# Weights' product first, and MoE blocks of 512 tokens in place of 384

## The reference

```python
# attention: q, k, v (2, 8, 768, 64), centroids (8, 16, 64)
q_assign = argmax(normalised q . normalised centroids); k_assign likewise
scores = where(q_assign == k_assign, scale * q @ k.T, -1e9)
attn = softmax(scores);  x = (attn @ v) as 1536 tokens x 512
# first MoE: w1, w2 (512, 1024), w3 (1024, 1024), w_out (1024, 512)
x = ((x @ w1) * (x @ w2)) @ w3 @ w_out
# second MoE: w_in (512, 2048), w_out (2048, 512), alpha (2048)
h = x @ w_in;  out = (max(h, 0) + alpha * min(h, 0)) @ w_out
```

## Time and profile before

| | us |
|---|---|
| median of 3 runs | 791.84 |
| lowest, highest | 790.97, 792.37 |
| the profiled execution | 791.99 |
| its span, first to last instruction | 790.2 |
| TensorE busy in the span | 761.5 |
| VectorE busy | 428.7 |
| ScalarE busy | 336.3 |
| GpSimd busy | 189.4 |

### The profile page before, as it was taken

The page is one execution under the profiler, slowest core; times in us unless marked ns, Lnnn a source line. Parts: engine busy times, 40 slices in busy tenths (PEclk is TensorE's granted clock), DMA queues, the critical chain, the costliest instruction groups (busy, mean ns, idle before and its releaser), DMA issues.

```text
span 790.2 us, 12079 instructions
## 1 busy us (share of the span) xinstructions
PE 761.5 (96%) x4290; PEld 712.8 (90%) x4290; DVE 428.7 (54%) x704; ACT 336.3 (43%) x679; POOL 189.4 (24%) x210
## 2 busy tenths in 40 slices
PE   5999999999999998899999999999999999999998
PEld 4887998898899987899999999999999999999997
DVE  5224988889889887542212115467344434443442
ACT  5124988888889787532112114242111112112111
POOL 2120576867767875300000000000000000000000
PEclk9999999999999999999999999999999999999999
DMA  8833464565555322330000003231010001001001
GB/s 284 163 100 98 101 155 105 127 142 127 121 126 134 92 66 63 85 108 1 1 1 0 0 0 107 80 121 67 0 41 1 1 1 40 0 0 40 1 1 40
DMA packets 63577, 54.13 MB, mean 69 GB/s; under 512 B 31264, under 2 KB 51760, under 8 KB 63536
## 3 DMA queue, kind: packets, MB, share of 16 engines
q1 hardware_dynamic: 63536, 53.59, 26.3%
HBM read 31.50 MB, written 3.19 MB: 44 GB/s over the span
## 4 chain that ended last, share of the span: by engine, by line
PE 75%; POOL 15%; issue 5%; DVE 2%; ACT 2%; DMA 1%; POOLq 0%; SPq 0%; ACTq 0%; DVEq 0%
PE slot L575 57%; PE acc L575 14%; POOL xf L520 3%; PE slot L638 3%; POOL xf L516 2%; POOL xl L526 2%; POOL v L469 1%; POOL oh L495 1%; POOL v L465 1%; POOL c L487 1%; POOL c L488 1%; PE slot L689 1%; POOL c L493 1%; POOL c L485 1%; DMA qk<-in_k 1%
## 5 line engine op out<-in xcount | busy, mean ns | idle before, releaser
L575 PE MATMUL slot<-xh,w 128*128 128x384 f32 (+1 forms) x1024 | 277.0, 336 | 0.0
L575 PEld LDWEIGHTS slot<-xh,w 128*128 128x128 f32 x1024 | 186.8, 188 | 2.4
L575 PE MATMUL slot<-xl,w 128*128 (+1 forms) x512 | 172.3, 336 | 0.0
L1027 ACT CAST gh<-gf 128x384 fp32r<-128x384 f32 x64 | 32.9, 514 | 204.2 <-PE acc L575 178.2
L1127 DVE TENSOR_REDUCE nm<-slot 128x1 f32<-128x768 f32 x96 | 91.2, 950 | 22.7 <-PE slot L575 22.3
L1133 DVE TENSOR_TENSOR pl<-slot,ph 128x384 fp32r<-128x384 f32 x192 | 97.6, 550 | 10.6 <-ACT ph L900 10.4
L900 ACT CAST ph<-slot 128x384 fp32r<-128x384 f32 x192 | 83.6, 487 | 35.9 <-PE slot L638 35.4
L575 PEld LDWEIGHTS slot<-xl,w 128*128 128x128 f32 x512 | 96.0, 187 | 2.2
L892 ACT ACTIVATE pf<-slot,nm 128x768 f32<-128x768 f32 x96 | 87.9, 916 | 8.8 <-DVE nm L1127 8.7
L575 PE MATMUL slot<-k,q 96*128 96x384 f32 (+1 forms) x384 | 83.6, 339 | 1.7 <-DVE xl L1089 1.7
L638 PE MATMUL slot<-ident,pf 128*128 128x128 f32 x576 | 81.5, 275 | 2.0 <-DVE pl L1133 1.6
(11 more groups left out here) (121 smaller groups left out, 1113.0 us busy)
## 6 DMA issues: line engine op xcount, KB each, us to landing
stage<-in_moe_w SPq DMA_DIRECT2D x16, 256.0 KB, 3.1
stage<-in_moe_w_in SPq DMA_DIRECT2D x16, 256.0 KB, 2.7
stage<-in_moe_w_out SPq DMA_DIRECT2D x16, 256.0 KB, 3.0
qk<-in_q SPq DMA_DIRECT2D x16, 192.0 KB, 3.9
...
```

Of the source, the lines that this page charges most:

```text
L575: return nc.tensor.matmul(o, a, b, start=start, stop=stop)
L1027: copy(gh[j % 2][:, :], gf[j % 2][:, :]).then_inc(gh_done, 1)
```

## The change

There are two parts.

1. The start: w3's first tile and w_out's first half megabyte are loaded first, q, k and v after the weights. TensorE turns w3 tile 0 and multiplies it chunk by chunk as the parts arrive (`product_first` waits for each part by itself), and the transposes of q and k, and the cluster scores, stand between the product tiles. The loop over tiles is written out. cn and al are turned in the acc banks, not in slot 0. ACT and DVE follow in the same order.
2. The MoE stages: a block is 512 tokens (`TN`), so there are three blocks and four output tiles in each. abh and abl are rings of four features (`NAB`) in place of eight; `ab_hi` waits for layer 2 of four features before. wch and wcl are halves of one tile. xh and xl are laid out chunk, token. The loops over the middle block are unrolled.

```diff
@@ -29,8 +29,9 @@
-NB = B * S // HS
-TB = HS // P
+TN = 512
+NB = B * S // TN
+TB = TN // P
@@ -42,6 +43,7 @@
+NAB = 4
@@ -108,8 +110,8 @@
-        xh = sb("xh", [P, NB * KC * HS], F32R)
-        xl = sb("xl", [P, NB * KC * HS], F32R)
+        xh = sb("xh", [P, KC * B * S], F32R)
+        xl = sb("xl", [P, KC * B * S], F32R)
@@ -163,25 +165,25 @@
-        asb = [sb(f"asb{i}", [P, HS], F32, ff) for i in range(2)]
-        ab = [sb(f"ab{i}", [P, HS], F32, ff) for i in range(2)]
-        wch = sb("wch", [P, NF, DM], F32R, ff)
-        wcl = sb("wcl", [P, NF, DM], F32R, ff)
-        abh = sb("abh", [P, NF, HS], F32R, ff)
-        abl = sb("abl", [P, NF, HS], F32R, ff)
+        asb = [sb(f"asb{i}", [P, TN], F32, ff) for i in range(2)]
+        ab = [sb(f"ab{i}", [P, TN], F32, ff) for i in range(2)]
+        wcx = sb("wcx", [P, NF, 2, DM], F32R, ff)
+        wch, wcl = wcx[:, :, 0], wcx[:, :, 1]
+        abh = sb("abh", [P, NAB, TN], F32R, ff)
+        abl = sb("abl", [P, NAB, TN], F32R, ff)
...
-        gh = [sb(f"gh{i}", [P, HS], F32R) for i in range(2)]
-        gl = [sb(f"gl{i}", [P, HS], F32R) for i in range(2)]
-        neg = sb("neg", [P, HS])
-        gf = [sb(f"gf{i}", [P, HS]) for i in range(2)]
+        gh = [sb(f"gh{i}", [P, TN], F32R) for i in range(2)]
+        gl = [sb(f"gl{i}", [P, TN], F32R) for i in range(2)]
+        neg = sb("neg", [P, TN])
+        gf = [sb(f"gf{i}", [P, TN]) for i in range(2)]
...
-        xview = lambda x: x[:, :].rearrange("p (n c t) -> p n c t", n=NB, c=KC)
...
-        pairs = lambda x: x[:, :].rearrange("p (b h c i t) -> p b h c i t", b=B, h=2, c=2, i=2)
+        xview = lambda x: x[:, :].rearrange("p (c n t) -> p n c t", n=NB, c=KC)
...
+        pairs = lambda x: x[:, :].rearrange("p (c i b h t) -> p b h c i t", b=B, h=2, c=2, i=2)
@@ -363,30 +365,33 @@
-            load_qk(0, 0)
-            load_v(0, 0)
-            load_v(0, 1)
-            load_qk(0, 1)
+            load_w3(0, 0)
+            load_wo(0)
...
-            load_w3(0, 0)
+            load_wo(1)
...
-            for i in range(NWO):
+            for i in range(2, NWO):
...
+            load_qk(0, 0)
+            load_qk(0, 1)
+            for parity in range(2):
+                sp.wait_ge(w3_turned, parity + 1)
+                load_w3(4 + parity, parity)
+            load_v(0, 0)
+            load_v(0, 1)
...
-            for parity in range(2):
-                sp.wait_ge(w3_turned, parity + 1)
-                load_w3(4 + parity, parity)
+            sp.wait_ge(w3_turned, 5)
+            load_w3(6, 0)
...
+            sp.wait_ge(w3_turned, 6)
+            load_w3(7, 1)
...
-            for parity in range(2):
-                sp.wait_ge(w3_turned, 4 + parity + 1)
-                load_w3(6 + parity, parity)
@@ -611,6 +616,8 @@
+                elif c == 1:
+                    pe.wait_ge(w3_lo, NF)
@@ -673,17 +680,14 @@
-                s = 2 - parity
-                if isinstance(f, int) and f < 4:
-                    source = stage[parity] if f < 2 else early[NWO + parity]
-                    if f < 2:
-                        pe.wait_ge(ld_stage[parity], 16)
-                    else:
-                        pe.wait_ge(ld_early[NWO + parity], 16)
+                s = 1 + parity
+                if f in (2, 3):
+                    source = early[NWO + parity]
+                    pe.wait_ge(ld_early[NWO + parity], 16)
...
-                    pe.wait_ge(ld_stage[parity], 8 * (f - parity))
-                if not isinstance(f, int) or f >= 2:
+                    pe.wait_ge(ld_stage[parity], 16 * (f // 2 + 1) if f < 2 else 16 * (f // 2))
+                if f >= 2:
@@ -699,40 +703,57 @@
+            def product_first():
...
+                o = slot[0][:, 0, :]
+                pe.wait_ge(piece_hi, 1)
+                pe.wait_ge(w3_hi, 1)
+                for g in range(2):
+                    mm(o, w3h[:, 0, g, :], woh[:, g, :], g == 0, False)
+                pe.wait_ge(piece_lo, 1)
+                for g in range(2):
+                    mm(o, w3h[:, 0, g, :], wol[:, g, :], False, False)
+                pe.wait_ge(w3_lo, 1)
+                for g in range(2):
+                    mm(o, w3l[:, 0, g, :], woh[:, g, :], False, False)
...
             def product_tile(f, parity):
...
-            for j in range(2):
+            turn_w3(0, 0)
+            pe.wait_ge(setup_act, 1)
+            nc.tensor.transpose(acc[0:D, 0, 0:P], cn[:, :], ident[:, :])
+            pe.wait_ge(ld_al, 16)
+            nc.tensor.transpose(acc[:, 1, 0:NJ], al16[:, :], ident[0:NJ, 0:NJ]).then_inc(cen_turned, 1)
+            product_first()
+            pe.wait_ge(piece_lo, 2)
+            product_wc(0, (2, 3))
+            turn_w3(1, 1)
+            for i in range(2, NWO):
+                pe.wait_ge(piece_lo, i + 1)
+                product_wc(0, (2 * i, 2 * i + 1))
+            turn_w3(2, 0)
+            pe.wait_ge(w3_lo, 2)
+            product_wc(1, range(NF // 2))
+            pe.wait_ge(table_done, 2)
+            for half in range(2):
+                turned(0, 0, half, True)
+            product_wc(1, range(NF // 2, NF))
+            for f in range(2, NF - 2):
+                turn_w3(f + 1, (f + 1) % 2)
                 for half in range(2):
-                    turned(0, j, half, True)
-            pe.wait_ge(setup_act, 1)
-            nc.tensor.transpose(slot[0][0:D, 0, 0:P], cn[:, :], ident[:, :])
-            pe.wait_ge(ld_al, 16)
-            nc.tensor.transpose(slot[0][:, 1, 0:NJ], al16[:, :], ident[0:NJ, 0:NJ]).then_inc(cen_turned, 1)
-            turn_w3(0, 0)
-            turn_w3(1, 1)
-            pe.wait_ge(table_done, 2)
-            for i in range(NWO):
-                pe.wait_ge(piece_lo, i + 1)
-                for f in range(2):
-                    if i == 0:
-                        pe.wait_ge(w3_lo, f + 1)
-                    product_wc(f, (2 * i, 2 * i + 1))
-            turn_w3(2, 0)
-            turn_w3(3, 1)
-            for half in range(2):
-                cluster(0, 0, half, True)
-            with pe.Fori(2, NF // 2) as i:
-                product_tile(2 * i - 2, 0)
-                turn_w3(2 * i, 0)
-                product_tile(2 * i - 1, 1)
-                turn_w3(2 * i + 1, 1)
-            for half in range(2):
-                turned(0, 2, half, True)
-            pe.wait_ge(w3_lo, NF)
+                    if f == 2:
+                        turned(0, 1, half, True)
+                    elif f == 3:
+                        cluster(0, 0, half, True)
+                    elif f == 5:
+                        turned(0, 2, half, True)
+                product_tile(f, f % 2)
+            turn_w3(NF - 1, 1)
+            pe.wait_ge(w3_lo, NF - 1)
             for c in range(LEAD):
@@ -751,7 +772,7 @@
-                    o = bank[2 * (f % 2) + w][:, 0:HS]
+                    o = bank[2 * (f % 2) + w]
@@ -768,10 +789,10 @@
                 for m in range(KC):
-                    o, cols = bank[4 + m][:, 0:HS], slice(m * P, (m + 1) * P)
-                    mm(o, wch[:, f, cols], abh[:, f, :], f == 0, False)
-                    mm(o, wch[:, f, cols], abl[:, f, :], False, False)
-                    last = mm(o, wcl[:, f, cols], abh[:, f, :], False, f == NF - 1)
+                    o, cols = bank[4 + m], slice(m * P, (m + 1) * P)
+                    mm(o, wch[:, f, cols], abh[:, f % NAB, :], f == 0, False)
+                    mm(o, wch[:, f, cols], abl[:, f % NAB, :], False, False)
+                    last = mm(o, wcl[:, f, cols], abh[:, f % NAB, :], False, f == NF - 1)
@@ -797,8 +818,7 @@
-            with pe.Fori(1, NB - 1) as n:
-                block1(n, False, False)
+            block1(1, False, False)
@@ -926,24 +945,26 @@
-            for j in range(2):
-                for half in range(2):
-                    operands_hi(0, j, half, True)
+            wo_hi(0)
...
-            wo_hi(0)
+            wo_hi(1)
+            wo_hi(2)
...
-            for i in range(1, NWO):
-                wo_hi(i)
-            for f in range(2):
-                w3_hi_part(2 + f, f)
-                wc_copy(f, f)
-            with act.Fori(2, NF // 2) as i:
-                wc_copy(2 * i - 2, 0)
-                w3_hi_part(2 * i, 0)
-                wc_copy(2 * i - 1, 1)
-                w3_hi_part(2 * i + 1, 1)
+            wo_hi(3)
+            w3_hi_part(2, 0)
+            wc_copy(0, 0)
...
-                operands_hi(0, 2, half, True)
+                operands_hi(0, 0, half, True)
+            w3_hi_part(3, 1)
+            for half in range(2):
+                operands_hi(0, 1, half, True)
+            wc_copy(1, 1)
+            for f in range(2, NF - 2):
+                w3_hi_part(f + 2, f % 2)
+                if f == 4:
+                    for half in range(2):
+                        operands_hi(0, 2, half, True)
+                wc_copy(f, f % 2)
@@ -967,22 +988,24 @@
             def a_out(n, f):
...
-                copy(asb[f % 2][:, :], bank[2 * (f % 2)][:, 0:HS]).then_inc(asb_done, 1)
```

(64 more changed lines are left out.)

32 lines of the change are left out of this document (15 added, 17 removed).

## The result

The changed kernel took 788.31 us (median of 7 runs, 786.77 to 788.67), the kernel before, on the same chip, 792.37 (790.97 to 796.23); the ratio is 0.9933, with a 95% interval of [0.9911, 0.9955]. The profiled execution took 788.31 around a span of 786.5, against 791.99 and 790.2. So it became faster by about 4 us, where 12.4 were forecast, and the time lies above the range.

What follows compares the result with a forecast made beforehand. TensorE, busy 96% of 790.2 us, was taken as the bound. Matmuls 8.5, start 3.5 and seam 0.4 sum to 12.4 us, so 791.84 becomes 779.4; own bounds 777 to 781.5, stretched by rivals to 775.5 to 784.

Steps and rivals of the forecast that it cites:

- The matmul term: MoE stages: 480 fewer matmuls through 512-token blocks save their fixed cost, 8.5 us, bounds 6.5 to 9.5.
- at the change of shape inside a unit: Second MoE: 0.035 us per unit beyond its matmuls' sum arises where column counts change, and goes when all are 512.
- Rival (c): MoE stages: a matmul's fixed part isn't saved; first MoE gains 0, second 2.2, giving 785.7 us; chance 0.04.
- The estimate in the prediction from the Trainium skill: MoE matmuls: by the gap rule, 480 x 2.5 ns = 1.2 us saved in place of 8.5, giving 786.7 us.
- The start: Weights loaded first let TensorE begin earlier; first score at 57.0 instead of 60.54, gain 3.5 us, ends 0 and 5.5.
- The masks: Before the first score: their transfers end by about 54 us, slack 3 us, so they are hidden.
- Rival (a): The new start gives nothing, masks late or TensorE waiting piece by piece; 782.9 us; chance 0.15.
- The seam: Between attention and first layer 2: TensorE's wait shrinks from 2.40 to about 2.0, 0.4 us gained; bounds 2.5 gained, 2 lost.
- the shift should hold: From the first score on: order is unchanged, so the time gained before it should be kept; ends 0 and 5.5 us.
- Evictions, ring, layout: MoE stages: longer evictions, the four-feature ring and new layouts stay covered by TensorE's work; cost 0.
- (b): A rival: new start gives 5.5 us and the wait before the first layer 2 closes; 775.9 us; chance 0.09.

Runs made afterwards that it cites:

- matmuls alone: Only TensorE matmuls, nothing of the reference computed, operand addresses varied: at 512 columns 226.6 to 227.6 ns with starts agreeing by 256 bytes, 232.4 to 233.3 otherwise.
- al first: The changed kernel with the 64-byte tile al allocated ahead of xh and xl: 779.10 us, ratio 0.9826 to the kernel before.
- al first on the kernel before: The kernel before, blocks of 384, with only al allocated ahead of xh: 794.37 us against 791.53 for the kernel before, ratio 1.0037.
- (21, 24, 26) on al first: The changed kernel with al ahead of xh and xl, and w12's fourth piece moved from step 28 to behind abl of feature 1: 776.64 us.
- the start alone: The changed kernel with its new start but blocks of 384 tokens as in the kernel before: 789.07 us, ratio 0.9951 to the kernel before.

## Why the prediction was wrong

**The matmul term (8.5 us) failed; it measured 0.0.** The step was "both sizes pay 0.0135 us over it", and from it 24 x 36 x 0.227 and 48 x 24 x 0.227. The 0.227 is real, and it is what 36 matmuls alone pay, but only with operands whose starts agree by 256 bytes, as those of the product in the earlier trace rows do. Layers 1 and 3 have operands that don't, and pay 0.2333 at 512 columns: (576 + 576) x 0.0067 = 7.7 us, and the first five matmuls of each of the 72 layers 2 and 4 behind them together 0.02 us, 1.4 more. With the remainders made equal (al first) the term is 9.2 us, inside its bounds of 6.5 to 9.5. So the mechanism (fewer matmuls, less fixed cost) is right and the price was taken from a row of other operands.

**The trace of before held the warning, and the prediction explained it away.** In the earlier trace rows a unit's 3.48 us are 12 matmuls of layer 3 and 6 of 512 columns; less 6 x 0.227 that leaves 2.12 / 12 = 0.1765 for layer 3, against 5.21 / 30 = 0.1737 in the first MoE. The prediction saw the 0.035 us and put them "at the change of shape inside a unit, which should go when all are 512 wide". In fact all twelve paid 3 ns more. Nor would equal remainders have removed them: there the change of shape really does cost, 0.062 (al first on the kernel before).

**Rival (c), given 0.04, came nearest**: "as if 512 columns cost 0.1735 x 4/3 = 0.2313", first MoE 0 saved, second 2.2, 785.7 us. Measured were 0.2333, nothing saved in either (-0.3 and 0.3) and 788.3. Its only counter-evidence was the product's 0.227, the row with other operands. The estimate in the prediction from the Trainium skill (TensorE: Matmul & The Clock Gate, Back-to-back issue gap: N/2.4 + 2.5 ns) was 786.7, near the measured 788.3. But no run shows the 2.5 ns: over 213.3 ns for the columns (four times the 53.3 between the steps at 384 and 512) matmuls alone pay 13.4 at equal remainders and 20 at others. So the estimate came near by luck.

**The start (3.5 us) was right in its mechanism; the two profiled executions give 4.8 at the first score and 5.4 at step 22**, at its upper bound of 5.5, and 3.65 at the score against an old start without a fall of the clock. TensorE began product_first at 8.28 (forecast 9.0), had two tiles at 26.15 (26.2 to 28.1), and what stands behind took 29.6 us (29.9). The forecast lay midway between a fall of the clock behind the wait at 17.7 and none, and there was none: the clock is 1.00 from 18 to 20. That is one execution: in that of (21, 24, 26) on al first the clock did fall there, and its score came at 57.48. The masks were no wait, as reckoned. Rival (a) is excluded by the start alone, 3.3 us faster by medians.

**The seam (0.4 us) was right**: 2.40 to 2.00, with POOL's subtraction and w12_lo still together (2.10 us). But a cost of 2.0 us just ahead of it was missing: behind the two waits at steps 21 to 23, unchanged in length, the clock fell. Nine of the eleven profiled executions have this pair of waits; with the new start the clock fell behind it in five of six, with the old one in none of three. "From the score on, the program's order is as before, so the shift should hold" was true of the order and not of the clock. That the new start is the reason isn't shown: these are single executions, and no run changes this alone.

**Evictions, ring, layout (0)**: no wait before layer 2 or 4 inside the stages; right. By sums: 5.4 + 0.0 - 2.0 + 0.3 = 3.7 us against 12.4, where the 2.0 holds the seam's 0.4.

**Bounds.** Three of the prediction's ends are off by their own working: 9.5 us of the matmul term is 0.2265 a matmul (0.2262 would be 10.1), (b) with it is 791.84 - 16.9 = 774.9 for 775.5, and (a) with 6.5 is 784.9 for 784. The result lies outside either way.
